# GpSimd's low part of the last layer's weights in eight operations of 128 columns instead of one of 1024

## The reference

```python
# attention: q [2, 12288, 128], kv [2, 384, 32, 128] averaged over 4 x 4 cells -> 768 keys
kv_flat = kv_pool.reshape(B, -1, C) @ w_sr
k = v = kv_flat
a = softmax(scale * (q @ k.transpose(0, 2, 1)));  x = a @ v          # 24576 tokens of 128
# first expert layer: 8 experts, 128 -> 1024 -> 128
expert = argmax(x @ w_gate);  x = gate * (relu(x @ w1[e]) @ w2[e])
# last expert layer: the same form, with its own weights
logits = (x / |x|) @ (emb / |emb|).T / tau;  expert = argmax(logits)
out = gate * (relu(x @ w1[e]) @ w2[e])
```

## Time and profile before

| | us |
|---|---|
| median of 3 runs | 2044.62 (2043.77 to 2048.84) |
| the profiled execution | 2049.17 |
| its span in the profile | 2047.3 |
| TensorE (matmul) busy | 1889.5, 92% |
| VectorE busy | 1490.3, 73% |
| ScalarE busy | 1238.4, 60% |
| GpSimd busy | 799.9, 39% |

### The profile page before, as it was taken

One profiled execution on the slowest core, in us unless ns is written; L12 is line 12 of the kernel. 1 busy time (PEld: TensorE's weight loads), 2 busy tenths in 40 slices (PEclk: granted clock), 3 DMA queues, 4 the chain that ended last, 5 costly groups with the idle time before them and its releaser, 6 DMA issues. The chain is left out here.

```text
span 2047.3 us, 62392 instructions
## 1 busy us (share of the span) xinstructions
PE 1889.5 (92%) x16614; PEld 1641.2 (80%) x16615; DVE 1490.3 (73%) x3978; ACT 1238.4 (60%) x3079; POOL 799.9 (39%) x1132
## 2 busy tenths in 40 slices
PE   4799999999999995998898999999499999999998
PEld 3688887878778884877787788888399999999997
DVE  6568999868788874777777777777466666666666
ACT  1266666657677772666666666666255555555554
POOL 0003333323333333366666644554433333333333
PEclk9699999989999996999999999999699999999999
DMA  9403333212333312133332321111111111111110
GB/s 226 120 22 95 104 122 111 92 32 69 112 105 121 104 33 71 31 92 94 92 103 90 89 58 47 45 45 33 44 50 47 48 50 46 43 50 46 48 50 27
DMA packets 131599, 148.78 MB, mean 73 GB/s; under 512 B 33070, under 2 KB 102842, under 8 KB 131520
## 3 DMA queue, kind: packets, MB, share of 16 engines
q1 hardware_dynamic: 90944, 87.57, 15.9%
q0 software_dynamic: 19328, 38.19, 5.5%
q10 hardware_dynamic: 21248, 22.04, 3.5%
HBM read 90.41 MB, written 42.39 MB: 65 GB/s over the span
## 5 line engine op out<-in xcount | busy, mean ns | idle before, releaser
L1859 DVE SCALAR_TENSOR_TENSOR hT_l<-ps_hidden,hT_l 128x512 f16<-128x512 f32 x412 | 283.1, 689 | 183.5 <-ACT hT_l L1816 160.0
L1569 DVE SCALAR_TENSOR_TENSOR hT_l<-ps_hidden,hT_l 128x512 f16<-128x512 f32 x412 | 282.9, 687 | 161.4 <-ACT hT_l L1515 155.4
L1816 ACT ACTIVATE hT_l<-ps_hidden 128x512 f16<-128x512 f32 x412 | 239.9, 597 | 228.0 <-PE ps_hidden L1758 226.6
L1898 POOL DMA_INDIRECT out<-out_rows_l,out_slots_l x206 | 200.4, 973 | 379.7 <-DVE out_rows_l L1867 336.8
L625 POOL DMA_INDIRECT rows<-att_rows,att_slots x192 | 188.2, 980 | 397.2 <-ACT exps L970 345.5
L1515 ACT ACTIVATE hT_l<-ps_hidden 128x512 f16<-128x512 f32 x412 | 243.5, 595 | 164.0 <-PE ps_hidden L1448 104.6
L1448 PE MATMUL ps_hidden<-xT_l,W 128*128 128x256 f16 x2472 | 339.1, 274 | 1.1 <-DVE xT_l L1564 1.1
L1758 PE MATMUL ps_hidden<-xT_l,W 128*128 128x256 f16 x2472 | 339.0, 274 | 1.0 <-DVE xT_l L1845 1.0
L1462 PE MATMUL ps_y<-W,hT_l 128*128 x1648 | 308.0, 280 | 32.5 <-DVE hT_l L1569 32.0
L1772 PE MATMUL ps_y<-W,hT_l 128*128 x1648 | 293.7, 273 | 0.5 <-DVE hT_l L1859 0.5
L1239 POOL DMA_INDIRECT rows<-grp_rows,grp_slots x206 | 205.3, 997 | 181.4 <-ACT grp_rows L1187 80.6
(11 more groups left out here) (192 smaller groups left out, 3185.3 us busy)
## 6 DMA issues: line engine op xcount, KB each, us to landing
x_l<-rows SPq DMA_DIRECT2D x206, 130.0 KB, 2.1
w_chunk<-in_moe_w SPq DMA_DIRECT2D x48, 512.0 KB
kv_raw<-in_kv SPq DMA_DIRECT2D x16, 768.0 KB, 9.9
q<-in_q SPq DMA_DIRECT2D x48, 256.0 KB
W<-weight_parts SPq DMA_DIRECT2D x16, 512.0 KB, 3.5
w_chunk<-in_moe_w ACTq DMA_DIRECT2D x16, 512.0 KB
W<-weight_parts ACTq DMA_DIRECT2D x16, 512.0 KB
w_raw<-in_moe_w ACTq DMA_DIRECT2D x8, 512.0 KB, 11.0
```

The lines of the kernel that those rows point to most:

```text
L1569: nc.vector.scalar_tensor_tensor(out=hT[:, p, 1, :], in0=psH[:, (HP * h + p) % HB, :], scalar=0.0, in1=hT[:, p, 0, :], op0=ALU.max, op1=AL ...
L1816: nc.scalar.activation(hT[:, p, 0, :], psH[:, p, :], ACT.Relu).then_inc(h_high, 1)
L1859: nc.vector.scalar_tensor_tensor(out=hT[:, p, 1, :], in0=psH[:, p, :], scalar=0.0, in1=hT[:, p, 0, :], op0=ALU.max, op1=ALU.subtract).then ...
```

## The change

pool_low makes the low part in a loop over the FB = 8 blocks of P = 128 columns, each with a `tensor_tensor` of its own. The last of them raises the semaphore.

```diff
     def pool_low(self, pool, e, w):
         pool.wait_ge(self.high, e * 2 + (w + 1))
-        self.nc.gpsimd.tensor_tensor(self.parts[:, :, 1, :], self.raw.rearrange("p (b c) -> p b c", c=P),
-                                     self.parts[:, :, 0, :], ALU.subtract).then_inc(self.low, 1)
+        for b in range(FB):
+            last = self.nc.gpsimd.tensor_tensor(self.parts[:, b, 1, :], self.raw[:, b * P:(b + 1) * P],
+                                                self.parts[:, b, 0, :], ALU.subtract)
+        last.then_inc(self.low, 1)
```

## The result

The changed kernel took 2060.98 us (median of 6 runs, 2057.67 to 2063.26), the kernel before 2047.98 us beside it (6 runs, 2043.77 to 2049.77): a ratio of 1.0066, 95% interval 1.0051 to 1.0081. It is 13 us slower, where 25.5 us faster was forecast. The profiled execution took 2060.02 us. First the head of its page.

The account below looks back on a forecast made before the run. TensorE was taken to wait for VectorE, held off by GpSimd's low part: 16 x 1.69 = 27.0 us, less 1.5 us of new waits, gains 25.5. From the median 2044.62 that gives 2019.1 us; own range 2015 to 2025.

Parts of the forecast that it names:

- What bounds the kernel: First expert layer: GpSimd's low part holds off VectorE's grp_power, so TensorE waits 1.69 us, 16 times, 27.0 us.
- GpSimd's own time: Low part as eight operations on GpSimd: 0.40 us each, 3.26 us in all, ending 1.1 us later.
- grp_power: Sign on VectorE: under 0.6 us in the 16 groups with a chunk, in place of 2673 ns.
- VectorE: Deciding step: two-input operations wait only for the rest of one GpSimd operation, at most some 0.4 us each.
- rival A: VectorE is let in nowhere; grp_power waits for the last of eight: +18 us, 2062.2 us; chance 0.16.
- the next load: Placed chunk lands by 987.1, next load comes at 989.3 on the new schedule: hidden.
- rival C: Wait changes owner: ScalarE's blocked queue or its L248 holds TensorE as long; no change, 2044.6 us; chance 0.09.
- The slack at the placing DMA: ScalarE's queue: high_h(1) 0.6 us late against about 1.1 us of slack, so hidden, though not by much.
- The sum: Whole kernel: 27.0 us gained less 1.5 us of new short waits, 25.5 us faster.
- rival B: Part of the hold or ScalarE's block at the placing DMA comes back: 13.5 us gained, 2031 us; chance 0.13.

Follow-up runs that it names:

- e3: Kernel before with the low part cut to 8 columns of each block, GpSimd filling memory without reading for 2.1 us in all; 0.9851 of the kernel before, prompt signals.
- e8: Kernel before, one low operation, with grp_power and grp_slots moved behind low_h(3) on VectorE's queue; 0.9870 of the kernel before, 2003.59 us, prompt signals.
- e5: The changed kernel (eight operations) run again beside the kernel before, with prompt signals; ratio 0.9962.
- e2: Kernel before, one operation, with the placing DMA issued one block later, behind high_h(1); 0.9985 of the kernel before, prompt signals.
- e12: The changed kernel (eight operations) once more against the kernel before, prompt signals; ratio 0.9947.
- e7: Low part as sixteen operations of 64 columns, against the kernel before, prompt signals; ratio 1.0046.
- e6: Low part as four operations of 256 columns, against the kernel before, prompt signals; ratio 0.9888.
- e13: Repeat of e4, GpSimd filling memory for 3.1 us in place of most of the low part; 0.9873 of the kernel before, prompt signals.
- e4: Like e3 but with the filling lengthened to some 3.0 us; 0.9877 of the kernel before, prompt signals.
- e17: The same program as e13, in the late-signal condition; 1.0053 of the kernel before.
- e18: Four low operations of 256 columns, as e6, in the late-signal condition; 0.9978 of the kernel before.
- e11: Eight operations, grp_power and grp_slots behind low_h(3), placing DMA behind high_h(1); 1.0065 of the kernel before, late signals.

## Why the prediction was wrong

**Right.** *What bounds the kernel*: the hold costs about 25 us, shown from two sides by e3 (no reading) and e8 (nothing beside it, 27 us by its ratio). *GpSimd's own time*: 3.26 us forecast, 3.12 measured, (3.12 - 0.42) / 7 = 0.39 us apart for 0.40. *grp_power* under 0.6 us.

**The step that failed first: VectorE.** It said that whoever asks during the low part waits for the rest of one operation, at most 0.4 us, and put grp_slots and grp_lg there at that price. grp_lg came after the low part and wasn't held (0.25 us, as before). grp_slots takes 1.97 us, almost to the end of the last operation. The true sum with prompt signals is: TensorE waits 16.6 us before ps_y in e5 against 28.0 in e2, so 11.4 us gained of some 25; about 0.6 us in each group behind grp_slots is 9.4 of the 16.6. The other 7.2 stand behind L248. The ratios of e5 and e12 give 8 and 11 us. This is rival A's mechanism, though not at the operation where A put it: grp_power gets through, its successor does not. A's evidence had been that grp_power stood from before the low part through the step from the note into it; I weighed it against "the gaps between eight operations are many", for which no row spoke. The Trainium skill (SBUF — State Buffer, § SBUF: two separate sides) gives the pair to whoever starts first "for the whole instruction"; e7, with twelve boundaries inside one hold, says that the next instruction in a row can take it over. By the Trainium skill (GPSIMD Engine Reference, § 2.1 Instruction dispatch) GpSimd's cores go on to the next instruction each by itself, so that their gaps need not meet. That would fit, but no row shows the cores singly. Why the first boundary always lets grp_power through, and why the second of e6 lets grp_slots through in some groups, stays open.

**The step priced at nothing: the next load, "Hidden".** It compared the landing of the placed chunk with the next load and stopped there; what a later load does to ScalarE at L248 has no term in the sum. Only rival C names L248. ScalarE's wait there for GpSimd's scaled chunk went from 9.3 to 28.1 us, and TensorE's waits behind it from 2.2 to 17.4. With prompt signals the same step costs less: TensorE waits 7.2 us there in e5 and 5.9 in e13, against 1.8 in e2. No run moved the load by itself, so this is read from the traces; that each of these waits ends 2.41 us after L248's start, in every profile, ties it to L248.

**The slack at the placing DMA.** It counted 0.6 us of delay at high_h(1) against 1.1 us of slack, with "some 0.2 us of signalling". ScalarE waits 1.78 us there. With prompt signals that is hidden, as forecast: in e4 and e13 no wait of TensorE stands behind it. With late ones, up to 1.33 us each in the kernel before, 0.2 us of signalling was far too little, and the longer low part goes with signals 2 to 3 us late (after, e17, e18). The recorded runs and the profile that I read were both of the late condition. The trace showed it in the line of waits above, ScalarE's wait for ps_y, 34.6 us; in e2 there is no such line. I read past it because the engine named had long been done. (One wait shows little of it: the 0.37 us before 985.87 in the earlier trace rows.)

**The sum, then.** It put the gain of the hold at 27.0 us and the new waits at 1.5. In the recorded profiles the hold gave 17.6, and the new waits are 15.2 behind L248 and 13.0 among the late signals: 10.6 us lost, where TensorE's idle time grew by 10.5 and the runs by 13. With prompt signals the change gains 8 to 11 us, not far from rival B, part of the hold coming back at grp_slots, which put it at 13.5; the sign that was measured hangs on a condition of the signals that no term of the prediction had.

**What stays open.** How a longer low part turns late signals of 1.3 us into 2 to 3 us was not found; e11, with the block moved, has them as well (54 above 1.5 us). Nor was it found what makes signals late on one occasion and never on another.

## What to carry to other kernels

Cutting a GpSimd operation into pieces opens it to VectorE only at the start: a request made once a row of eight or sixteen ran waited for nearly all of it, and with four it got in early in 18 of 48 groups. Move VectorE's two-input operations out of its time instead, as in e8, which came to 0.984 to 0.987 of the time before in both conditions and adds no instruction. Before counting slack in an engine's queue, look in the waits for an engine named as late that had long been done: signalling cost over 1 us here and ate the slack. The line alone doesn't tell it (e4, with prompt signals, has it for the block at the placing DMA); the increments do. And follow a delayed load to the operation that needs its data, not only to the load.

## What the hardware showed that I had not expected

In the first expert layer TensorE's semaphore increments came within 0.02 us of the block's end in every profile of one condition (420 of 420 in e5 in 870 to 1195 us), and over 0.1 us late for 99 of 378 in the same program in the other, with a granted clock of 0.970 and 0.971: the clock doesn't show it. The kernel before takes 2031 to 2033 us in the one and 2048 to 2057 in the other, 0.7% to 1.3% apart, and the same edit is 0.996 or 1.007. A difference below 1% measured on one occasion need not hold on the next.

A GpSimd operation of the low part takes 2.14 us for 1024 columns, and in a row 0.39 us for each 128 and 0.26 us for each 64. By these two, (0.39 - 0.26) / 64 = 2.0 ns is a column and 0.13 us a start, an estimate; it gives 0.65 us for each 256, and e6 shows 0.63.
